# First MoE of an attention-MoE-MoE kernel: x prepared in pieces, weights split two tiles ahead, gates kept in PSUM, first weights loaded earlier

## What is computed

```python
# q, k, v: (4, 8, 576, 64)
scores = (q @ k.T) / 8
scores = where(scores >= max(scores) - tau, scores, -1e9)
attn = exp(scores - max(scores)); attn = attn / (sum(attn) + 1e-9)
x = (attn @ v) as (2304 tokens, 512)
# first MoE: w_a, w_b (512, 1536), w_out (1536, 512)
x = ((x @ w_a) * (x @ w_b)) @ w_out
# second MoE: w_in (512, 1024), w_out (1024, 512)
h = x @ w_in
sm = exp(h - max(h)) / (sum(exp(h - max(h))) + 1e-9)
out = layernorm(h * sm) * g_ln @ w_out
```

## Time and profile before

| | us |
|---|---|
| median of 3 runs (1033.87 to 1040.49) | 1037.77 |
| the profiled execution: its time | 1034.12 |
| its span, first to last instruction | 1032.3 |
| TensorE matmul busy in the span | 957.4 (93%) |
| VectorE busy | 797.3 (77%) |
| GpSimd busy | 632.0 (61%) |
| ScalarE busy | 506.1 (49%) |
| mean granted clock of TensorE | 0.983 |

### The profile page before, as it was taken

One profiled execution on the slowest core, in us unless ns is written; L12 is line 12 of the kernel. 1 busy time (PEld: TensorE's weight loads), 2 busy tenths in 40 slices (PEclk: granted clock), 3 DMA queues, 4 the chain that ended last, 5 costly groups with the idle time before them and its releaser, 6 DMA issues.

```text
span 1032.3 us, 19024 instructions
## 1 busy us (share of the span) xinstructions
PE 957.4 (93%) x6222; PEld 880.1 (85%) x6222; DVE 797.3 (77%) x1288; ACT 506.1 (49%) x823; POOL 632.0 (61%) x580
## 2 busy tenths in 40 slices
PE   5999999999997886999999989999999899999998
PEld 4999999999997886888888888888888777888886
DVE  6787788787884575788768777877798778888884
ACT  3777777777776434333433343334433454333332
POOL 2777777877776447566766676657566863444320
PEclk9999999999999897999999999999999899999999
DMA  6667666666642743111321132113211200000001
GB/s 177 149 162 169 152 164 157 162 161 159 149 122 79 225 143 83 62 63 63 100 67 61 65 92 75 63 46 117 87 63 41 82 1 21 30 30 21 20 21 41
DMA packets 55678, 96.68 MB, mean 94 GB/s; under 512 B 15576, under 2 KB 24408, under 8 KB 55632
## 3 DMA queue, kind: packets, MB, share of 16 engines
q1 hardware_dynamic: 55632, 96.10, 33.9%
HBM read 58.41 MB, written 5.32 MB: 62 GB/s over the span
## 4 chain that ended last, share of the span: by engine, by line
PE 52%; issue 19%; POOL 12%; DVE 11%; ACT 3%; DMA 1%; SPq 1%; POOLq 0%; DVEq 0%; ACTq 0%
PE PS L1599 12%; PE PS L1561 8%; PE PS L1563 8%; POOL w_raw L705 3%; POOL w_raw L708 3%; PE PS L1802 3%; PE PS L1804 3%; PE PS L1803 3%; PE PS L1745 3%; PE PS L1746 2%; PE PS L1747 2%; POOL w_raw L699 2%; DVE w_od_rolled L1190 2%; POOL w_raw L707 2%; PE PS L1626 2%
## 5 line engine op out<-in xcount | busy, mean ns | idle before, releaser
L648 POOL TENSOR_TENSOR p_lo<-prob,p_hi 128x576 fp32r<-128x576 f32 x144 | 207.8, 1445 | 50.2 <-ACT p_hi L832 48.3
L1626 PE MATMUL PS<-x_parts,w_parts 128*128 128x256 f32 x672 | 194.2, 289 | 30.8 <-DVE w_parts L1311 30.8
L1561 PE MATMUL PS<-ops 128*128 128x288 f32 x642 | 181.9, 305 | 14.3 <-DVE ops L1235 6.8
L1628 PE MATMUL PS<-x_parts,w_parts 128*128 128x256 f32 x672 | 192.5, 286 | 0.0
L1627 PE MATMUL PS<-x_parts,w_parts 128*128 128x256 f32 x672 | 192.5, 286 | 0.0
L1563 PE MATMUL PS<-ops 128*128 128x288 f32 x642 | 177.3, 298 | 0.0
L701 POOL TENSOR_TENSOR w_parts<-w_raw,w_parts 128x768 fp32r<-128x768 f32 x48 | 96.5, 2011 | 120.2 <-ACT w_parts L951 120.2
L1626 PEld LDWEIGHTS PS<-x_parts,w_parts 128*128 128x128 f32 x672 | 131.3, 195 | 35.8 <-issue 26.4
L1155 DVE TENSOR_REDUCE neg_max<-PS 128x1 f32<-128x576 f32 x144 | 108.4, 755 | 59.7 <-PE PS L1563 59.5
L1561 PEld LDWEIGHTS PS<-ops 128*128 128x128 f32 x642 | 122.4, 191 | 23.2 <-issue 12.2
L955 ACT ACTIVATE w_parts<-w_raw 128x1024 fp32r<-128x1024 f32 x48 | 50.9, 1061 | 180.5 <-POOL w_raw L708 180.5
(11 more groups left out here) (164 smaller groups left out, 2314.9 us busy)
## 6 DMA issues: line engine op xcount, KB each, us to landing
w_raw<-w_ab_dram SPq DMA_DIRECT2D x60, 512.0 KB, 3.3
qk_raw<-qkT_dram SPq DMA_DIRECT2D x32, 288.0 KB, 3.0
ops<-qk_hi SPq DMA_DIRECT2D x62, 144.0 KB
ops<-qk_hi SPq DMA_DIRECT2D x31, 288.0 KB
ops<-qk_lo SPq DMA_DIRECT2D x62, 144.0 KB
v_raw<-v_tiles_dram SPq DMA_DIRECT2D x32, 160.0 KB, 2.7
xT<-head_sb SPq DMA_DIRECT2D x32, 144.0 KB, 3.2
out_dram<-o_sb SPq DMA_DIRECT2D x18, 256.0 KB, 2.0
```

What stands on the lines that cost most here:

```text
L648: pool.tensor_tensor(p_lo[:, s, :], prob[:, s, :], p_hi[:, r, :].bitcast(F32), ALU.subtract).then_inc(p_lo_done, 1)
L1561: pe.matmul(ps[:, b, 0:HALF], weights[0][:, r, own], moving[0][:, r, cols], start=(n == 0), stop=False)
L1626: pe.matmul(up_ps(bank, half), w[:, 0, :], x[:, 0, :], start=(k == 0), stop=False)
L1628: ins = pe.matmul(up_ps(bank, half), w[:, 1, :], x[:, 0, :], start=False, stop=(k == 1))
```

## The change

1. **Loads.** Tile 0 of the first weights is loaded one pair of heads earlier; tiles 1 and 2, and tiles 0 to 2 of the second matrix, within the last two pairs, ahead of the moves of the last head.
2. **Pass 0.** `high_w(1)` and `low_w(1)` move into the last pair of attention. All low parts of pass 0's weights are VectorE's (a semaphore of their own, `w_first_lo`). The normalisation and sums for pass 1 are GpSimd's (`normalize_first`, `sum_first`), once the reciprocals are there.
3. **Passes 1 to 4.** ScalarE's `high_blocks` runs two tiles ahead instead of one, behind `high_sums` of the next tile and ahead of the gates. VectorE's x work is one operation a tile: a normalisation on each of tiles 3 to 6, a sum on each of 7 to 10. The two gate halves are left in PSUM, first halves of banks 2 and 3, and `up` waits for their low part ahead of bank 2 instead of two waits on `up_done`.
4. **Last pass.** The win pieces are dealt one to a tile; `low_win` of T1, B22 and T4 move behind the pass, between the first sums of the second MoE.

The diff, cut to its core:

```diff
+        gates_ps = PS[:, 2:4, 0:H]
+        def in_halves(g):
+            return g.rearrange("p (b n) -> p b n", b=2)
...
 # SyncE, step of attention
-                if isinstance(i, int) and 2 * i + e == PAIRS - 2:
-                    load_w(0)
+                if isinstance(i, int):
+                    if 2 * i + e == PAIRS - 3:
+                        load_w(0)
+                    if 2 * i + e == PAIRS - 2:
+                        load_wo(0)
+                        load_w(1)
+                    if 2 * i + e == PAIRS - 1:
+                        load_wo(1)
+                        load_w(2)
+                        load_wo(2)
...
-            load_w(1)
-            load_wo(0)
+            load_w(3)
             move_head(last, ROLL - 1)
             spread_sums(PAIRS - 1, 1)
-            load_w(2)
-            load_wo(1)
+            load_wo(3)
             store_inverse(PAIRS - 1, 1)
...
 # GpSimd
+            def normalize_first():
+                for j in range(ROLL):
+                    pool.wait_ge(head_moved[j], 16 * (heads // ROLL))
+                pool.wait_ge(inverse_in, INVERSE_LOADS * 2)
+                for k in range(NK):
+                    x = xT[:, k, tokens(1)]
+                    pool.tensor_tensor(x, x, inverse_x[:, k, :], ALU.mult).then_inc(x_normed, 1)
+            def sum_first():
...
+                pool.tensor_tensor(s1, a21, a22, ALU.add).then_inc(x_sum_done, 1)
+                pool.tensor_tensor(s3, a11, a21, ALU.subtract).then_inc(x_sum_done, 1)
+                pool.tensor_tensor(s2, s1, a11, ALU.subtract).then_inc(x_sum_done, 1)
+                pool.tensor_tensor(s4, a12, s2, ALU.subtract).then_inc(x_sum_done, 1)
...
-            for f in range(2, NF):
-                low_w(f)
+            normalize_first()
+            sum_first()
             prepare(1, 0)
...
 # ScalarE
-                elif k == NK:
-                    high_w(0)
+                elif k in (NK, NK + 2):
+                    high_w((k - NK) // 2)
...
             def later_step(c, f):
-                if not last:
-                    high_blocks(nc_, nf)
                 copy_product(c, f)
-                if not last:
-                    high_sums(nc_, nf)
-                if f == NF - 1 and not last:
+                if f + 1 < NF:
+                    high_sums(c, f + 1)
+                elif not final:
+                    high_sums(c + 1, 0)
+                if f + 2 < NF:
+                    high_blocks(c, f + 2)
+                elif f + 2 == NF and not final:
+                    high_blocks(c + 1, 0)
+                if f == NF - 1 and not final:
                     high_x_block(c + 1, 0)
-                act.wait_ge(up_done, UPS * (NF * c + f) + UPS)
-                high_gate(c, f)
+                high_gates(c, f)
-                if f == NF - 1 and not last:
+                if f == NF - 1 and not final:
                     for part in range(1, 4):
                         high_x_block(c + 1, part)
+                    high_blocks(c + 1, 1)
...
 # ScalarE, pass 0
             for f in range(NF):
+                first_gate(f)
+                if f == NF - 2:
+                    high_blocks(1, 0)
                 if f == NF - 1:
-                    high_blocks(1, 0)
-                first_gate(f)
-                if f == NF - 1:
-                    high_sums(1, 0)
                     high_x_block(1, 0)
-                act.wait_ge(g_done, f + 1)
-                high_gate(0, f)
+                high_gate(f)
                 if f + 2 < NF:
                     high_w(f + 2)
                     high_wo(f + 2)
-            for part in range(1, 4):
-                high_x_block(1, part)
+            high_x_block(1, 1)
+            high_sums(1, 0)
+            high_x_block(1, 2)
+            high_x_block(1, 3)
+            high_blocks(1, 1)
...
 # ScalarE, last pass
-                for b in {2: (B11,), 3: (B21,), 5: (T3,), 6: (T2,), 10: (T1,), 11: (B22, T4)}.get(f, ()):
+                for b in {2: (B11,), 4: (B21,), 6: (T3,), 8: (T2,), 10: (T1,)}.get(f, ()):
                     high_win(b)
...
             copy_first(0)
+            high_win(B22)
+            high_win(T4)
...
 # VectorE
-                        if s == 4:
-                            low_w(0)
+                        if s in (4, 6):
+                            low_w((s - 4) // 2)
...
+            def low_gates(c, f):
                 dve.wait_ge(g_hi_done, NF * c + f + 1)
-                dve.tensor_tensor(g_part(1, c, f), gate[:, 0:width(c)], g_part(0, c, f).bitcast(F32),
+                dve.tensor_tensor(in_halves(g_part(1, c, f)), gates_ps, in_halves(g_part(0, c, f)).bitcast(F32),
                                   ALU.subtract).then_inc(g_lo_done, 1)
...
-                done(dve.tensor_tensor(first, first, up_ps(2, 1), ALU.mult))
+                done(dve.tensor_tensor(up_ps(2, 0), first, up_ps(2, 1), ALU.mult))
...
-                done(dve.tensor_tensor(second, second, up_ps(3, 0), ALU.mult))
+                done(dve.tensor_tensor(up_ps(3, 0), second, up_ps(3, 0), ALU.mult))
...
-                if f == 4 and not last:
-                    normalize(c + 1, inverse_x)
-                if f == 6 and not last:
-                    dve.wait_ge(xs_lo_done, 2 * c)
-                    sum_x(c + 1)
+                if 3 <= f < 3 + NK and not final:
+                    normalize(c + 1, inverse_x, (f - 3,))
+                if 3 + NK <= f < 7 + NK and not final:
+                    sum_x(c + 1, f - 3 - NK)
...
 # VectorE, behind the last pass
-            early_sums(0)
+            low_win(T1)
+            early_sums(0, (0, 1))
+            low_win(B22)
+            early_sums(0, (2,))
+            low_win(T4)
             late_sums(0)
...
 # TensorE, up(c, f)
-                pe.wait_ge(up_done, UPS * (n - 1) + 7)
+                pe.wait_ge(g_lo_done, n)
...
-                pe.wait_ge(up_done, UPS * (n - 1) + UPS)
```

More of the change, by code:

```diff
@@ L562, in load_w @@
                 else:
-                    at_least(sp, w_lo_done, before + 1)
+                    at_least(sp, w_first_lo, before + 1)
                 sp.dma_start(w_raw[:, f % RAW, :, :].rearrange("p b n -> p (b n)"), w_ab[f]).then_inc(w_raw_in[f % RAW], 16)
@@ L686, in _ @@
             low_probs(last, 1, SLOTS - 1)
[L688 to L692, removed]
+            def normalize_first():
[6 more added lines that the diff above has]
+            def sum_first():
+                (a11, a12), (a21, a22) = ([xT[:, 2 * j:2 * j + 2, tokens(1, i)] for j in range(2)] for i in range(2))
+                s2, s3, s1, s4 = (x_sums[:, b] for b in range(4))
+                pool.wait_ge(x_normed, NK * 2)
+                pool.tensor_tensor(s1, a21, a22, ALU.add).then_inc(x_sum_done, 1)
+                pool.tensor_tensor(s3, a11, a21, ALU.subtract).then_inc(x_sum_done, 1)
+                pool.wait_ge(x_sum_done, 1)
+                pool.tensor_tensor(s2, s1, a11, ALU.subtract).then_inc(x_sum_done, 1)
+                pool.wait_ge(x_sum_done, 3)
+                pool.tensor_tensor(s4, a12, s2, ALU.subtract).then_inc(x_sum_done, 1)
             def prepare(c, f):
@@ L724, in _ @@
                 prepare(c + 1, 0)
[L725 removed]
+            low_x_sums(LAST_CHUNK)
             for f in range(1, NF):
@@ L935, in y_out, with high_gate, high_gates @@
                     act.activation(xT[:, m, tokens(c)], PS[:, 4 + m, 0:width(c)], ACT.Copy).then_inc(y_out_act, 1)
-            def high_gate(c, f):
+            def high_gate(f):
+                at_least(act, y_done, f - 1)
+                act.wait_ge(g_done, f + 1)
+                act.activation(g_part(0, 0, f), gate[:, 0:H], ACT.Copy).then_inc(g_hi_done, 1)
+            def high_gates(c, f):
                 if not (isinstance(c, int) and c == LAST_CHUNK and f >= NF - 2):
-                    at_least(act, y_done, NF * c + f - 1)
-                act.activation(g_part(0, c, f), gate[:, 0:width(c)], ACT.Copy).then_inc(g_hi_done, 1)
+                    act.wait_ge(y_done, NF * c + f - 1)
+                act.wait_ge(up_done, UPS * (NF * c + f) + UPS)
+                act.activation(in_halves(g_part(0, c, f)), gates_ps, ACT.Copy).then_inc(g_hi_done, 1)
             def first_gate(f):
@@ L1337, in later_step @@
             def later_step(c, f):
-                last = isinstance(c, int) and c == LAST_CHUNK
+                final = isinstance(c, int) and c == LAST_CHUNK
                 products(c, f)
@@ L1341, in later_step @@
                     low_sums(c, f + 1)
-                    low_gate(c, f)
-                elif not last:
+                    low_gates(c, f)
+                elif not final:
+                    low_x_block(c + 1, 0)
+                    low_gates(c, f)
                     low_sums(c + 1, 0)
-                    low_x_block(c + 1, 0)
-                    low_gate(c, f)
                     low_x_block(c + 1, 1)
                 else:
-                    low_gate(c, f)
-                if f == 4 and not last:
```

(44 more changed lines are left out.)

59 lines of the change are left out of this document (34 added, 25 removed).

## The result

The changed kernel takes 1008.89 us (median of 4 runs, 1005.52 to 1010.75) for 1037.55, the median of the kernel before with a fourth run added: a ratio of 0.972 (0.968 to 0.977). The forecast was 1004. Its profiled execution has a span of 1008.7 us for 1032.3, 23.6 less, and the same mean clock, 0.983.

The account below looks back on a forecast made before the run. TensorE was taken as full except for pauses, waits in pass 0 and slow clock. 1034.1 profiled, terms -9.9 - 1.5 - 3.9 - 18.8 - 3.9 + 4 = -34.0, plus 3.7 to the median: 1004 us, range 990 to 1027.

Parts of the forecast that it names:

- Pass 0: First MoE pass up to bank 1 of up(1,1): 68.0 us against 87.5; with 0.7 lost in attention, -18.8 us.
- the alternation with GpSimd: Middle of pass 0: GpSimd's eight x operations alternate with three of VectorE's per tile, losing 2.9 us (0 to 8).
- The lock at L1311: Passes 1 to 4: VectorE's L1311 waits out GpSimd's L701; 0.05 us lost a tile, pause between tiles 10 and 11 2.8.
- Pause between tiles 0 and 1: Start of each pass: VectorE goes first, so TensorE's pause becomes 2.3 us, 2.7 before.
- x spread: Passes, tiles 3 to 10: x work one piece a tile; both 2.3 us pauses go, at worst 2.4 us a pass lost.
- Last pass: Last pass of 87.2 us: win pieces one a tile, slow clock gone; -3.9 us (0 to -5).
- Into the second MoE: After the last pass: two low_win move behind the first hidden sum, T4's wait of 0.4 remains; -3.9 us (-1 to -4).
- Clock: First MoE: ten stretches of slow clock after pauses stay or come, +4 us (0 to 12).
- A: Rival, chance 0.2: only pass 0 and the ends pay, the passes win nothing; 1018 us (1011 to 1025).
- C: Rival, chance 0.05: L701 starts just ahead of L1311 in every tile, blocking it; slower, 1052 us.
- B: Rival, chance 0.1: after eight of ten pauses the clock stays at half for 6.8 us, +27 for +4; 1027 us.
- D: Rival, chance 0.15: pass 0's pauses are half of those forecast and the clock stays up; 994 us.

Follow-up runs that it names:

- short low part: Changed kernel with GpSimd's low part L728 for one plain block in place of three, same order and waits: 995.7 us, ratio 0.957.
- spread-only kernel: Kernel before with only x's normalisation and sums for passes 2 to 4 as one VectorE operation a tile, tiles 3 to 10: 1025.4 us, ratio 0.987.
- pass-0-only kernel: Kernel before with only the earlier loads and pass 0 of the change; passes 1 to 4 as before: 1017.9 us, ratio 0.979.
- kernel with the sums before the gate: Changed kernel with the weight sums' low halves moved ahead of the gate and half of x's low sums on VectorE: 987.3 us, ratio 0.951.

## Why the prediction was right, and where not

The changed kernel is faster for the reasons that the forecast gave, pass 0 above all, and the total is 5 us off. But several steps missed, and their misses partly cancel. The profiled executions differ by -23.6 us in span where the sum has -34.0, 10.4 us apart. Slow clock makes 9 of these, the way into the second MoE 3, the three passes at full clock 3 and attention's end 1; pass 0 and the last pass came out better by 4 and 2 at full clock. Then the two executions happened to lie badly: the changed one 1.9 us over the median of its kernel (1010.75), the one of before 3.4 under (1034.1). By the medians the change is worth 28.7 us, and that is how 10 us become 5. That part is luck. By its steps:

- **Pass 0** ("68.0 against 87.5"): 67.3, with 6.8 us at clock 0.50 that cost about 3 and that the sum did not book here. `down(0)` began 1.2 us after `up(1)` (1.5), the alternation with GpSimd cost 1 to 1.5 us (2.9 forecast), the last gate waits 3.4 (2.7), bank 1 of `up(1,1)` 2.8 (3.6). The 0.6 and 0.9 did not come. The first copy of pass 1 is at 389.0, as the signs asked ("near 390"). Attention's end lost 1.5, not 0.7; no run takes that apart.
- **The lock at L1311** ("0 to 0.3 us lost a tile; I take 0.05"): 0.1; tiles of 7.87 for 7.78. "so that pause, 1.8 before, is 2.8": 2.8. The short low part shows that the lock is the cause.
- **Pause between tiles 0 and 1** ("I take 2.3"): 3.1. The step failed. It has VectorE's L1311 go first as something new, but it did so before (below: 1.22 us long, not locked), so there was nothing to win. And L1359, now behind the gates, falls on the start of GpSimd's x operations, which take 5.91 us for 5.33; everything behind them, to TensorE, takes 7.2 us as before. A pass is 100.2 and not 99.3, -2.4 and not -3.3.

```profile
505.34 5.33 POOL L713 TENSOR_TENSOR x_parts<-x_sums,x_parts 128x1024 fp32r<-128x1024 f32 x2 [3.83 <-ACT x_parts L972]
516.64 1.22 DVE L1311 TENSOR_TENSOR w_parts<-w_raw,w_parts 128x1024 fp32r<-128x1024 f32 x1 [0.79 <-ACT w_parts L955]
...
487.55 1.22 DVE L1359 TENSOR_TENSOR w_parts<-w_raw,w_parts 128x1024 fp32r<-128x1024 f32 x1
487.93 5.91 POOL L740 TENSOR_TENSOR x_parts<-x_sums,x_parts 128x1024 fp32r<-128x1024 f32 x2 [7.43 <-ACT x_parts L1007]
```

  The first two lines are of the kernel before, the others of the changed one.

- **x spread** ("both pauses of 2.3 us go"): right, 4.1 us a pass with the lock not added. "If each piece met an L701 ... 2.4 us a pass": each did in the spread-only kernel, and it cost nothing, so the bound of the range was too careful.
- **Last pass** ("-3.9"): -4.2, with one stretch of slow clock still in it. No run takes the win pieces alone.
- **Into the second MoE** ("-3.9"): -0.8. TensorE starts the downs 3.2 us sooner counted from the last `up`, but 2.5 of these are given back at the first transposition, which waits 2.6 us for ScalarE's copy of y (L962). That copy stands in ScalarE's queue behind `high_wout`, and `high_wout` waits for a DMA, in both kernels (before, then changed):

```profile
820.37 0.72 ACT L1052 ACTIVATE wout_raw<-wout_raw,gain 128x512 f32<-128x512 f32 x1 [3.48 <-DMA wout_raw<-w_out_dram]
...
797.61 0.72 ACT L1090 ACTIVATE wout_raw<-wout_raw,gain 128x512 f32<-128x512 f32 x1 [3.65 <-DMA wout_raw<-w_out_dram]
```

  SyncE issues that load 0.3 us after the last `up` (`sp.wait_ge(ab_done, NF * NCH)`), so ScalarE can begin 8.6 us after it before and 8.7 in the changed kernel, and the transposition starts 25.4 and 25.1 us after it (25.0 to 25.8 in eleven of the twelve traces, 26.8 in the spread-only one). I followed the wait for T4 and not the next one, which hangs on this load. In the pass-0-only kernel, whose way into the second MoE is that of before, TensorE comes 3.2 us later and that wait is 0.4 us. No run issues the load earlier.
- **Clock** ("+4"): the step mis-sized most. From 382 to 710 us the changed kernel shows 6.8 + 6.8 + five times 3.4 us at the level of 1.2 GHz, seven stretches behind eight pauses of 2.8 to 3.6 us: 30.7 us in all, which cost some 13. My +4 was called half of what passes 0 to 4 had, but the earlier trace rows gives them some 14 (12% of 78.5 us, and 1.5, and 3.4), so half would have been 7. And one of the signs of being wrong, "if slow clock follows most pauses", did come true.

The rivals: A (passes give nothing) is refuted by the passes at full clock, though the profile alone looks like it. C's mechanism exists and was worth 7.6 us, not 48. B, the clock, is the nearest to what is missing. D had pass 0's pauses at half: they are 9 us for the forecast's 12.6; but its clock did not stay up.

## What to carry to other kernels

Before moving an operation earlier on GpSimd, look which VectorE operation with two SBUF inputs it will then be ahead of: being early cost more here than being late. Take a change of several parts apart: of 29 us over two thirds were one pass, one part cost 8 us, and two did nothing that the runs show. Where a consumer's input is ready early, try the consumer early as well: the new order of one VectorE operation was worth as much as the whole spread (13.5 us each). And when a wait goes, look for the next one behind it: 2.5 of 3.2 us went to a copy whose time hung on a load issued at the last `up`.

## What the runs showed of the hardware

The granted clock followed the length of TensorE's pauses, from one matmul to the next. In the first MoE of the twelve traces 64 pauses were 1.1 to 2.0 us long, and behind none of them did the clock fall. It fell to 0.50, the level of 1.2 GHz, at or just behind 22 of the 37 pauses of 2.2 to 2.8 us, 26 of the 36 of 2.8 to 3.5, and 15 of the 16 of 3.6 and more, for 3.4 or 6.8 us each time. Why one pause of 2.3 us had a fall and the next had none stays open. The kernel with the sums before the gate has pauses of 1.1 to 1.5 us in its passes and no fall in them:

```profile
PEclk9999999999999998999999999999999999999999
```

Only the fall at the 3.6 us pause at the end of pass 0 is left. A fall of 3.4 us cost 1.5 us, so a pause of 3 us costs near 4.5 when it comes, and one of 1.5 costs 1.5.
